# Layer 1's pair chain reordered on ScalarE and VectorE, a fifth seven-product pair per tile, and other first waits in layer 2

## The reference

```python
qn = q / (norm(q, axis=1) + 1e-06); kn = k / (norm(k, axis=1) + 1e-06)
a = softmax(kn.T @ qn / tau)
x = v @ a
h = x @ w_in1;  g = where(h > 0, h, exp(min(h, 0)) - 1);  y1 = g @ w_out1
h = y1 @ w_in2; g = h / (1 + exp(-h));                    out = g @ w_out2
```

## Time and profile before

| | |
|---|---|
| median of three runs | 1004.13 us (1003.95 to 1005.28) |
| the profiled execution | 1004.19 us, span 1002.4 us |
| TensorE (PE) busy | 996.2 us, 99% |
| its weight loads (PEld) | 897.5 us, 90% |
| VectorE (DVE) busy | 834.8 us, 83% |
| ScalarE (ACT) busy | 717.0 us, 72% |
| the chain that ended last | PE 98%, DVE 1%, issue 1% |
| granted TensorE clock | 1.00 (2.4 GHz) to the end of the work |

### The profile page before, as it was taken

The page is one execution under the profiler, slowest core; times in us unless marked ns, Lnnn a source line. Parts: engine busy times, 40 slices in busy tenths (PEclk is TensorE's granted clock), DMA queues, the critical chain, the costliest instruction groups (busy, mean ns, idle before and its releaser), DMA issues.

```text
span 1002.4 us, 14378 instructions
## 1 busy us (share of the span) xinstructions
PE 996.2 (99%) x5157; PEld 897.5 (90%) x5157; DVE 834.8 (83%) x991; ACT 717.0 (72%) x1103; POOL 10.2 (1%) x11
## 2 busy tenths in 40 slices
PE   9999999999999999999999999999999999999998
PEld 8888989899899899999999888888888888888997
DVE  7779898889888988888796777887888887888886
ACT  6789878788787787877786666666666666666664
POOL 0300000000000000000000000000000000000000
PEclk9999999999999999999999999999999999999999
DMA  9913221312312123030003433334236235334333
GB/s 349 377 20 74 43 64 27 90 48 43 85 53 44 48 43 87 37 82 22 1 19 147 134 110 117 111 86 183 95 81 203 73 94 173 104 94 131 111 100 90
DMA packets 137403, 97.52 MB, mean 97 GB/s; under 512 B 114176, under 2 KB 120832, under 8 KB 137344
## 3 DMA queue, kind: packets, MB, share of 16 engines
q1 hardware_dynamic: 136736, 96.26, 32.0%
q10 hardware_dynamic: 608, 0.49, 0.2%
HBM read 77.07 MB, written 19.66 MB: 97 GB/s over the span
## 4 chain that ended last, share of the span: by engine, by line
PE 98%; DVE 1%; issue 1%; ACT 0%; DMA 0%; DVEq 0%; ACTq 0%
PE banks L1351 49%; PE banks L1554 21%; PE banks L1466 13%; PE banks L1494 10%; PE banks L1361 4%; DMA early_qk<-k 0%; PE banks L1588 0%; PE banks L1463 0%; PE banks L1596 0%; ACT g_pair L876 0%; ACT g_pair_parts L892 0%; DVE m_tile L1330 0%; DVE y_sums L1100 0%; DVE g_forms L1220 0%; PE banks L1394 0%
## 5 line engine op out<-in xcount | busy, mean ns | idle before, releaser
L1351 PE MATMUL banks<-x_parts,w_in_parts 128*128 128x512 f32 (+1 forms) x1152 | 274.8, 375 | 0.2 <-ACT g_pair L876 0.2
L1351 PE MATMUL banks<-xT_parts,a_w_in 128*128 128x512 f32 (+1 forms) x1152 | 259.3, 375 | 0.1
L1351 PEld LDWEIGHTS banks<-x_parts,w_in_parts 128*128 128x128 f32 x1152 | 215.6, 189 | 28.9 <-ACT g_pair L876 1.2
L1554 PE MATMUL banks<-g_pair_parts,w_forms 128*128 128x512 f32 (+1 forms) x987 | 239.3, 375 | 0.0
L1351 PEld LDWEIGHTS banks<-xT_parts,a_w_in 128*128 128x128 f32 x1152 | 214.4, 189 | 24.4 <-issue 0.5
L1554 PEld LDWEIGHTS banks<-g_pair_parts,w_forms 128*128 128x128 f32 x987 | 186.5, 189 | 22.1
L876 ACT ACTIVATE g_pair<-banks 128x512 f32<-128x512 f32 (+1 forms) x192 | 112.8, 588 | 125.8 <-PE banks L1351 118.8
L1466 PE MATMUL banks<-g_parts,w_out_parts 128*128 128x512 f32 (+1 forms) x613 | 140.6, 375 | 0.0
L1038 DVE SCALAR_TENSOR_TENSOR g_raw<-g_raw,banks 128x1024 f32<-128x1024 f32 (+1 forms) x96 | 114.9, 1197 | 29.2 <-ACT g_raw L769 28.9
L764 ACT ACTIVATE g_raw<-banks 128x512 f32<-128x512 f32 (+1 forms) x192 | 110.4, 575 | 37.7 <-PE banks L1351 37.5
L1233 DVE TENSOR_TENSOR g_pair_parts<-g_forms,g_pair_parts 128x1024 fp32r<-128x1024 f32 (+1 forms) x96 | 115.1, 1200 | 21.9 <-ACT g_pair_parts L885 21.7
(11 more groups left out here) (112 smaller groups left out, 829.7 us busy)
## 6 DMA issues: line engine op xcount, KB each, us to landing
w_forms<-w_forms SPq DMA_DIRECT2D x48, 896.0 KB, 4.6
w_forms<-w_out_forms SPq DMA_DIRECT2D x8, 896.0 KB, 4.2
early_qk<-q SPq DMA_DIRECT2D x23, 256.0 KB, 7.6
early_qk<-k SPq DMA_DIRECT2D x22, 256.0 KB, 7.9
y_raw<-y_sums SPq DMA_DIRECT2D x40, 128.0 KB, 2.1
x_parts<-y_raw SPq DMA_DIRECT2D x10, 512.0 KB, 5.9
out<-out_tile SPq DMA_DIRECT2D x40, 128.0 KB, 2.7
v_in<-v SPq DMA_DIRECT2D x36, 128.0 KB, 3.5
```

The lines of the kernel that those rows point to most:

```text
L1351: mm = pe.matmul(dst, lhsT, rhs, start=first and n == 0, stop=last and n == len(todo) - 1)
L1554: mm = pe.matmul(m_banks[m][:, 0:u.n], ring[k % N_RING][:, form, x, :], by_turns(gp2[k % 2][:, y, operand, 0:u.n]), start=k == 0 and part ...
```

## The change

It does four things.

- VectorE makes g of pair k in slot k instead of slot k+1, and puts behind it the low parts of pair k-1 (for a seven-product pair only those of its sums; its sums and plain low parts are now made at the end of the pair's own slot). ScalarE puts all high parts of pair k-1 that need g ahead of ReLU of pair k, and the high parts of the sums behind the last exp.
- `ONE_WINO` gets pair 4 as a fifth seven-product pair; the forms' tensor has room for five blocks and the block order changes.
- Side work moves to other slots: `form_sums` to 6, `form_hi` to 7, `form_lo` stays in 7, the y rows to slot 1, the v steps to 1, 2 and 6; `y_sums` is split, its first sum in slot 7 and the rest in the next tile's slot 0.
- In layer 2's first tile the y rows of tile 11 go behind the second pair's sums and the first pair's plain low parts, and the third pair's first up waits for the fifth SiLU instead of the eighth.

The core of the diff:

```diff
-SLOT_FORM_SUM, SLOT_FORM_HI, SLOT_FORM_LO = 5, 5, 7
-SLOT_V_TURN, SLOT_V_HI, SLOTS_V_LO = 2, 2, (5, 7)
-SLOT_ROWS = 2
-COPY_LAG, SUM_LAG = 2, 3
-SLOTS_FIRST_X_HI, SLOTS_FIRST_X_LO = (1, 3), (2, 5)
+SLOT_FORM_SUM, SLOT_FORM_HI, SLOT_FORM_LO = 6, 7, 7
+SLOT_V_TURN, SLOT_V_HI, SLOT_V_LO = 1, 2, 6
+SLOT_FIRST_Y, SLOT_ROWS = 2, 1
+SLOT_COPY, SLOT_SUM_U2, SLOT_SUM_U3 = 7, 7, 0
+SLOTS_FIRST_X_HI, SLOTS_FIRST_X_LO = (0, 5), (1, 6)
-ONE_WINO = (0, 2, 3, 5)
-BLOCKS_OF_PAIR = (0, 1, 2, 4, 3, 6, 5, 7)
+ONE_WINO = (0, 2, 3, 4, 5)
+BLOCKS_OF_PAIR = (0, 5, 1, 2, 3, 4, 6, 7)
+N_ONE = len(ONE_WINO)
-        forms1 = place("w_out1_forms", [P, 4, PAIRS // 2, 2, P], F32R)
+        forms1 = place("w_out1_forms", [P, 4, N_ONE, 2, P], F32R)
...
@@ ScalarE, slot_one
                 if is_wino:
                     one_plain_hi(*back)
-                relu(ph, k, 0)
-                if is_wino:
-                    one_sums_hi(*back)
                 elif back:
                     normal_hi(*back)
+                relu(ph, k, 0)
                 exp(ph, k, 0)
                 relu(ph, k, 1)
                 exp(ph, k, 1)
-                if ph.wino and k == ph.wino[-1] + COPY_LAG:
+                if is_wino:
+                    one_sums_hi(*back)
+                if ph.wino and k == SLOT_COPY:
                     one_copy(ph)
...
@@ VectorE, slot_one
                 back = shifted(ph, k, 1, PAIRS)
-                if ph.tile > 1 and k == SLOT_ROWS:
-                    y_row(ph.before, 0)
-                if back:
-                    one_g(*back)
-                if ph.tile > 1 and k == SLOT_ROWS:
-                    y_row(ph.before, 1)
+                if ph.tile > 1 and k == SLOT_SUM_U3:
+                    y_sum_u3(ph.before)
+                one_g(ph, k)
+                if back and back[1] in back[0].wino:
+                    one_sums_lo(*back)
+                elif back:
+                    normal_lo(*back)
+                if ph.wino and k == SLOT_SUM_U2:
+                    y_sum_u2(ph)
+                for c in range(CB):
+                    if ph.tile > 1 and k == SLOT_ROWS:
+                        y_row(ph.before, c)
...
-                if back and back[1] in back[0].wino:
-                    one_sums(*back)
-                    one_plain_lo(*back)
-                    one_sums_lo(*back)
-                elif back:
-                    normal_lo(*back)
+                if k in ph.wino:
+                    one_sums(ph, k)
+                    one_plain_lo(ph, k)
...
@@ VectorE, tile of layer 2
                     if u is TWO[0] and k == 0:
-                        one_g(ONE[-1], PAIRS - 1)
-                        y_sums(ONE[-1])
                         normal_lo(ONE[-1], PAIRS - 1)
+                        y_sum_u3(ONE[-1])
...
-                    first = u is TWO[0] and k == 1
-                    if first:
-                        plain_lo(*back)
-                        for c in range(CB):
-                            y_row(ONE[-1], c)
                     pair_sums(u, k, 0)
                     pair_sums(u, k, 1)
-                    if back and not first:
+                    if back:
                         plain_lo(*back)
+                    for c in range(CB):
+                        if u is TWO[0] and k == 1:
+                            y_row(ONE[-1], c)
...
@@ TensorE, pair_up
+                elif u is TWO[0] and k == LAG_PAIRS and i == 0:
+                    pe.wait_ge(u_act, up_of(u, 1, FIRST_H.index(0, 4) - 4) + 1)
```

More of the change, by code:

```diff
@@ L156, in build @@
         cursor[0] = at_end
-        form1_raw = place("w_out1_form_sums", [P, 4, PAIRS // 2, 2, P], F32, at_forms1)
+        form1_raw = place("w_out1_form_sums", [P, 4, N_ONE, 2, P], F32, at_forms1)
         form_stage = place("form_stage", [P, 2, CB, P], F32, at_xb)
@@ L353, in build, with wino_before @@
         wino_index = lambda ph, k: ph.wino_before + ph.wino.index(k)
+        def wino_before(ph, k):
+            i = ph.wino.index(k)
+            return (ph, ph.wino[i - 1]) if i else (ph.before, ph.before.wino[-1])
         def quarters(ph, x):
@@ L835, in slot_one @@
             def slot_one(ph, k):
-                if ph.tile == 1 and k == SLOT_ROWS:
-                    first_y_copy(ONE[0])
                 back = shifted(ph, k, 1, PAIRS)
                 is_wino = back is not None and back[1] in back[0].wino
+                if ph.tile == 1 and k == SLOT_FIRST_Y:
+                    first_y_copy(ONE[0])
                 if is_wino:
                     one_plain_hi(*back)
-                relu(ph, k, 0)
-                if is_wino:
-                    one_sums_hi(*back)
                 elif back:
                     normal_hi(*back)
+                relu(ph, k, 0)
                 exp(ph, k, 0)
@@ L1073, in one_sums_lo, with y_sum_u2, y_sum_u3 @@
                                   ALU.subtract).then_inc(u_lo, 1)
-            def y_sums(ph):
-                n = Y_SUMS * (ph.tile - 1)
-                half = lambda b, i: bank[b][:, i * ph.n // 2:(i + 1) * ph.n // 2]
+            def y_sum_u2(ph):
                 dve.wait_ge(m1_copy, ph.tile)
                 dve.wait_ge(p1_down, one_pair(ph, ph.wino[-1]) + 1)
-                dve.tensor_tensor(half_plain(y_sum(ph, Y_U2)), half_turned(half(*one_m[M6])),
+                b, half = one_m[M6]
+                dve.tensor_tensor(half_plain(y_sum(ph, Y_U2)), half_turned(bank[b][:, half * ph.n // 2:(half + 1) * ph.n // 2]),
                                   half_plain(y_sum(ph, Y_P1)), ALU.add).then_inc(c1_sum, 1)
+            def y_sum_u3(ph):
+                n = Y_SUMS * (ph.tile - 1)
+                b, half = one_m[M7]
                 dve.wait_ge(c1_sum, n + 1)
-                dve.tensor_tensor(half_plain(y_sum(ph, Y_U3)), half_turned(half(*one_m[M7])),
+                dve.tensor_tensor(half_plain(y_sum(ph, Y_U3)), half_turned(bank[b][:, half * ph.n // 2:(half + 1) * ph.n // 2]),
                                   half_plain(y_sum(ph, Y_U2)), ALU.add).then_inc(c1_sum, 1)
@@ L1179, in slot_one @@
                 for c in range(CB):
-                    if ph.tile and ph.v_next and k == SLOTS_V_LO[c]:
+                    if ph.tile and ph.v_next and k == SLOT_V_LO:
                         vT_lo(*ph.v_next, c)
@@ L1491, in wino_down @@
                             pe.wait_ge(c1_sum, Y_SUMS * (ph.tile - 2) + 2)
-                    weights = forms1[:, form, BLOCKS_OF_PAIR[k] // 2, x, :] if form <= S4 else \
+                    weights = forms1[:, form, BLOCKS_OF_PAIR[k], x, :] if form <= S4 else \
                         wout1[:, f_block(ph, k, form != A11), x, (form == A22) * P:(form == A22) * P + P]
```

6 lines of the change are left out of this document (2 added, 4 removed).

## The result

The changed kernel takes 1008.70 us (median of six runs, 1007.96 to 1010.21); the kernel before takes 1004.75 on the same chip (1003.95 to 1005.28). The ratio is 1.0042, with a 95% interval from 1.0029 to 1.0055: slower by some 4.0 us, where 1004.6 with a range to 1007.0 was forecast. The profiled execution took 1007.96 us, 3.77 us more than the profiled execution before; the spans, 1006.16 and 1002.37 us, differ by 3.80.

What follows compares the result with a forecast made beforehand. TensorE, the only engine without slack, was taken to bound the kernel. From 1004.19 us, conversions -2.13, the opening of tile 0 +3.2 and layer 2's entry -0.65 gave 1004.6 us, range 1003.2 to 1007.0.

Steps and rivals of the forecast that it cites:

- The opening gap: Tile 0, before the first down step: TensorE waits 3.10 us for pair 0's low parts, cost +3.2 us with restart.
- rival (a): Tile 0's opening does not stall because something supplies the first low parts earlier: 1001.4 us, chance 0.11.
- Rival (c): The clock falls in tile 0's opening wait and the recovery costs about 2 us: 1006.6 us, chance 0.08.
- Later slots of tile 0: After the opening, low parts come 0.5 us or more ahead of TensorE, so the stall occurs once.
- The conversions: Fifth seven-product pair: saves 0.25 us in each of tiles 1 to 9, loses 0.06 on each of two; sum -2.13 us.
- The narrow matmuls: On the two tiles of 448 columns, narrowing from 256 to 224 columns buys nothing: 0.111 us per matmul either way.
- The chain keeps up: From one g to the next takes 4.80 us, against TensorE's 4.93 for a seven-product slot, so lag is worked off.
- VectorE's load: A conversion adds 2.5 us of VectorE work per tile: 38.7 us busy against TensorE's 40.2, which fits.
- The tight spot: Each form tile, low parts of its last pair: ready 0.30 us before TensorE wants them, no stall taken.
- The entry of layer 2: Layer 2's first tile: earlier SiLU wait and moved y rows gain 0.65 us, bounds 0.3 and 0.85.

Runs made afterwards that it cites:

- the kernel with the weights first and the small matmuls: Changed kernel with the weights' low parts ahead of g in tile 0, plus 11 idle 128-column matmuls before the first down step's wait: 1005.56 us.
- the kernel with four pairs: Changed kernel with four seven-product pairs (0, 2, 3, 5) instead of five, new order and the rest kept: 1010.46 us, ratio 1.0061.
- the one with the extra copy: Changed kernel with tile 0 in the old order, plus one more 128x512 ScalarE copy in form_hi in tiles 1 to 8: 1005.22 us, ratio 1.0005.
- the one with the weights first: Changed kernel with a weight piece's low parts moved ahead of g on VectorE in tile 0: 1007.17 us, ratio 1.0022.

## Why the prediction was wrong where it was

The forecast sum was 1004.6 us and the profiled execution took 1007.96, 3.4 us more. Two terms that the sum had at nothing make 3.0 of it: 1.5 for the clock and 1.46 for late low parts behind the weights' load. The rest is 0.26 later in layer 2 and small pieces. The median, 1008.70, lies another 0.7 us higher.

**The opening gap: right.** Low parts were to end at 69.57 and TensorE to start at 69.67, 3.10 us late. VectorE's rows:

```profile
67.20 1.22 DVE L1044 SCALAR_TENSOR_TENSOR g_raw<-g_raw,banks 128x1024 f32<-128x1024 f32 x1 [3.48 <-ACT g_raw L775]
68.34 1.22 DVE L1049 TENSOR_TENSOR g_parts<-g_raw,g_parts 128x1024 fp32r<-128x1024 f32 x1
```

They end at 69.56, TensorE starts at 69.61, 3.08 us late. With the restart that is 3.19 where 3.2 stood in the sum. So rival (a), an opening without a stall, did not come.

**The clock: wrong in its chance.** Rival (c) named the mechanism and gave 2 us and a chance of 0.08. It was the likeliest case: the fall came in all eleven runs of the changed kernel and cost 1.5 us here (1.61 less the restart), 1.65 where nothing else follows. The step that failed is the reading of the earlier trace rows: more than 3 us of rest before a fall shows that so much is enough, not that so much is needed. The row bounds the needed rest from above only, and the prediction took it as a bound from below for a gap of 2.9 us. Other ends of the span show how little one such row says. In the kernel with the weights first and the small matmuls, the last matmul ends at 999.04 and the clock falls 1.8 us later (windows as above):

```profile
999.04:1000.80 1.76, 0.00 (x0) 0.00 (x0) 0.69 (x1) 0.10 (x1) 0.00 (x0) 1.00 0.82 232
1000.90:1003.00 2.10, 0.00 (x0) 0.00 (x0) 0.00 (x0) 0.00 (x0) 0.00 (x0) 0.50 0.50 145
```

In the kernel before it fell 3.3 us behind the last matmul. The Trainium skill's page "TensorE: Matmul & The Clock Gate", section "HAM oscillation — how this bites in real kernels", has such a fall in the middle of a kernel behind each of its waits for a load, which it puts at some 3 to 5 us. The runs agree that it happens there, and show it behind a slightly shorter wait: 2.91 us idle and half the clock after it. The size, taken from the earlier trace rows as 2 us for sixteen short matmuls, was a little high. (The profile prints a granted clock of 1.00 over those first matmuls too; the prediction read their level from their pace.)

**Later slots of tile 0: wrong.** "Later slots of tile 0 have low parts 0.5 us or more ahead" holds up to the down step of pair 5, where they end 1.0 to 2.0 us ahead. The down steps of tile 0's own pairs 6 and 7, which TensorE does between the first ups of tile 1, find them late: at 102.75 and at 108.19, for 0.82 us with the restarts. A third wait, at 118.95, belongs to tile 1 (0.65 with its restart). The counting stopped at the engines, while the same reordering moved the weights' low parts. It left out the queue behind them: low parts, staging buffer, load, ScalarE. With the weights' low parts moved ahead of g all three are gone, which makes 1.46 us. The prediction looked at SP's transfers only at the entry of layer 2, where they cost nothing.

**The two missed terms aren't simply added.** In the changed kernel the clock's 1.5 us lie in the shadow of the weight waits: taking the fall away alone gains nothing in the trace up to tile 2 (83.26 against 82.97, one execution each). Taking the waits away alone gives 1.34, both together 3.0 (profiled executions of 1006.62 and 1004.96 us).

**The conversions: right.** 0.25 in each of tiles 1 to 9 (one tile has a hiccup of 0.09; in the changed kernel itself tile 1's gain is hidden by the waits), a loss of 0.08 in each of tiles 10 and 11 for the forecast 0.06. The narrow matmuls gained nothing from 224 columns, as the row had it.

**The chain keeps up, as forecast; VectorE's load was put too high.** The cycle was put at 4.80 us by the chain and repeats every 4.92, which is TensorE's own pace of 4.93; so it is shown that the chain fits, and the 4.80 itself is not measured. VectorE is busy 37.30 in 40 us, against 38.7 in 40.2 forecast. A conversion does add 2.5 us (851.6 less 824.3 in the kernel with four pairs, over eleven tiles), but the new order by itself takes 10.5 us off the whole (834.8 to 824.3), which wasn't in the sum. It isn't less work: the lengths of VectorE's records add up to 872.7 and 872.1 us. With fewer waits between them, more of its instructions overlap the one before, and the busy time counts an overlap once.

**The tight spot: right.** g of the next tile's first pair was forecast 5.11 us after its first matmul and starts 5.09 after it (302.28 to 307.37); the low parts end at 309.73, TensorE wants them at 310.05:

```profile
302.28 2.76 PE L1358 MATMUL banks<-xT_parts,a_w_in 128*128 128x512 f32 x12
307.37 1.22 DVE L1044 SCALAR_TENSOR_TENSOR g_raw<-g_raw,banks 128x1024 f32<-128x1024 f32 x1 [1.00 <-ACT g_raw L775]
308.51 1.22 DVE L1049 TENSOR_TENSOR g_parts<-g_raw,g_parts 128x1024 fp32r<-128x1024 f32 x1
310.05 2.75 PE L1473 MATMUL banks<-g_parts,w_out_parts 128*128 128x512 f32 x12
```

The slack is 0.32 for the forecast 0.30, in every one of these tiles.

**The entry of layer 2: right.** 0.66 for 0.65, also in the kernel before with that change alone.

**What stays open.** Between 706 and 711 us of layer 2 the changed kernel loses 0.23 of the 0.26 us, behind a SiLU that waited 0.49 for a sum. The 0.26 stand in every kernel with five pairs, in the old order too, except the one with the extra copy, and in none of the three with four (the kernel before among them). No experiment addressed it.

## What to carry to other kernels

An order that keeps the steady state free of waits also says how far the chain must be ahead when it is entered; at a ramp-up, with the bounding engine right behind, that lead is paid in full, so the first slots want an order of their own (here, with the weights' low parts put back as well, it turned +4.0 us into -2.1). When a step is moved, follow what it frees through the DMA to its next use, not only the instructions behind it on its engine. And a wait of TensorE of about 3 us should be priced with a fall of the clock behind it: a row that shows a fall after a longer rest is no evidence that a shorter one is safe. Nor is the rest of 1.80 us that went without a fall, since at the end of another run the clock fell 1.8 us behind the last matmul.

## What the runs showed of the hardware

The granted clock fell to half for over 3 us behind 2.91 us of idle time in 26 of 27 timed runs of the three kernels with this gap (by their mean clocks; the changed kernel, the one with four pairs, the one with the weights first), and didn't in the traces with 1.80 us and 0.46 us of idle time in its place. In the four traces with the gap the fall came between 0.3 us before TensorE took up work again and 1.3 us after it. At the ends of the spans it came 1.8 us behind the last matmul in one trace and 3.3 us in another. A float32 matmul of 128 columns into the unused bank stands in the trace as two matmuls of 0.11 us each.
